# Shared sums of the second transform, mixing ahead of their reading in the drain, and an inverse root under the value products: one change to a fused attention, gated-MLP and mixer kernel

## What is computed

```
scores = q @ k.T / 8 ; thresh = max(scores) - tau
attn   = exp(scores - max), zero where scores < thresh, over its row sum
x      = attn @ v                                  (B, S, 512)

xk, xr = mu*x + (1-mu)*x_prev                      (two mixes with the row before)
k      = relu(xk @ w_k) (512->1024);  v = k*k @ w_v (1024->512)
x      = sigmoid(xr @ w_r) * v

u      = x + real(fft over channels of fft over the sequence of x)
un     = (u - mean(u)) / sqrt(var(u) + 1e-6)
out    = u + relu(un @ w_ch1) @ w_ch2              (512->2048->512)
```

## Time and profile before

| | us |
|---|---|
| median of 3 runs | 1114.38 |
| lowest, highest | 1113.59, 1114.43 |
| the profiled execution | 1115.46 |
| its span, first to last instruction | 1113.7 |

### The profile page before, as it was taken

One profiled execution on the slowest core, in us unless ns is written; L12 is line 12 of the kernel. 1 busy time (PEld: TensorE's weight loads), 2 busy tenths in 40 slices (PEclk: granted clock), 3 DMA queues, 4 the chain that ended last, 5 costly groups with the idle time before them and its releaser, 6 DMA issues.

```text
span 1113.7 us, 18462 instructions
## 1 busy us (share of the span) xinstructions
PE 1078.5 (97%) x7088; PEld 1012.4 (91%) x7088; DVE 551.7 (50%) x1081; ACT 512.7 (46%) x1250; POOL 420.0 (38%) x360
## 2 busy tenths in 40 slices
PE   7999999999999999999998999999999999999998
PEld 6899999998899998899997998888888888888998
DVE  7988764466565566565563655334114123223211
ACT  5979876646675646775644643221111111111110
POOL 5887653533663433763413445351111111111000
PEclk9989999999899999999999899999999999999999
DMA  8635111042121032121022207300200200200000
GB/s 237 176 98 170 37 43 34 24 140 53 65 56 35 23 104 89 66 57 34 2 71 77 105 1 287 122 1 1 69 1 1 69 1 1 68 1 1 35 1 33
DMA packets 37251, 69.30 MB, mean 62 GB/s; under 512 B 4134, under 2 KB 18604, under 8 KB 36140
## 3 DMA queue, kind: packets, MB, share of 16 engines
q1 hardware_dynamic: 36860, 67.80, 19.5%
q10 hardware_dynamic: 304, 0.33, 0.1%
HBM read 55.84 MB, written 12.28 MB: 61 GB/s over the span
## 4 chain that ended last, share of the span: by engine, by line
PE 82%; POOL 6%; DVE 4%; issue 3%; ACT 3%; DMA 0%; SPq 0%; DVEq 0%; POOLq 0%; ACTq 0%
PE PB L731 20%; PE PB L733 19%; PE PB L732 19%; PE PB L788 10%; PE PB L758 6%; PE PB L771 6%; POOL mix_l L630 1%; DVE probs L1284 1%; POOL x2T L662 1%; DVE neg_s L1270 1%; POOL q_hl L579 1%; POOL x2T L663 1%; POOL k_lo L571 1%; ACT exps L1019 1%; POOL fold_l L651 1%
## 5 line engine op out<-in xcount | busy, mean ns | idle before, releaser
L1228 ACT ACTIVATE h_hi<-PB 128x464 fp32r<-128x464 f32 (+1 forms) x80 | 44.5, 556 | 335.6 <-PE PB L733 335.6
L1461 DVE SCALAR_TENSOR_TENSOR h_lo<-PB,h_hi 128x464 fp32r<-128x464 f32 (+1 forms) x80 | 51.0, 638 | 264.0 <-ACT h_hi L1228 264.0
L788 PE MATMUL PB<-v_sb,probsT 128*128 128x64 f32 (+1 forms) x1440 | 180.2, 273 | 0.0
L788 PEld LDWEIGHTS PB<-v_sb,probsT 128*128 128x128 f32 x1440 | 175.1, 195 | 0.0
L1028 ACT ACTIVATE probsT<-PB 128x384 f32<-128x384 f32 (+1 forms) x288 | 109.5, 433 | 84.5 <-PE PB L771 83.5
L1284 DVE SCALAR_TENSOR_TENSOR probs<-neg_s,thresh,exps 128x576 f32<-128x576 f32 x144 | 145.7, 1012 | 0.3 <-PE PB L771 0.3
L1270 DVE TENSOR_SCALAR_CACHE_REDUCE neg_s<-PB,taus 128x576 f32<-128x576 f32 x144 | 117.1, 814 | 42.4 <-PE PB L758 38.1
L731 PE MATMUL PB<-un_h,w1h 128*128 128x464 f32 (+1 forms) x320 | 121.7, 380 | 0.0
L733 PE MATMUL PB<-un_h,w1l 128*128 128x464 f32 (+1 forms) x320 | 118.9, 371 | 0.0
L732 PE MATMUL PB<-h_lo,w2h 128*128 128x464 f32 (+1 forms) x320 | 118.8, 371 | 0.0
L731 PE MATMUL PB<-h_hi,w2h 128*128 128x464 f32 (+1 forms) x320 | 118.8, 371 | 0.0
(11 more groups left out here) (154 smaller groups left out, 2398.6 us busy)
## 6 DMA issues: line engine op xcount, KB each, us to landing
q_raw<-qT_dram SPq DMA_DIRECT2D x62, 160.0 KB, 3.2
k_raw<-kT_dram SPq DMA_DIRECT2D x64, 144.0 KB, 3.2
w_raw<-w_dram SPq DMA_DIRECT2D x8, 1024.0 KB, 9.3
cs<-cs_scr SPq DMA_DIRECT2D x4, 1740.0 KB, 8.0
u_scr<-x2T SPq DMA_DIRECT2D x4, 1152.0 KB, 5.2
cd<-cd_scr SPq DMA_DIRECT2D x4, 1032.0 KB
v_sb<-v_dram SPq DMA_DIRECT2D x16, 256.0 KB, 2.9
u_in<-u_scr SPq DMA_DIRECT2D x4, 928.0 KB, 6.1
```

Of the source, the lines that this page charges most:

```text
L788: last = nc.tensor.matmul(bank(6 + p)[:, i * DH:i * DH + width], probsT[:, n % 2, kt * P128:(kt + 1) * P128], v_sb[:, kt, pair % 2, p * DH ...
L1461: nc.vector.scalar_tensor_tensor(h_lo[:, ft % 3, 0:w], bank(4 + ft % 3)[:, 0:w], 0.0, h_hi[:, ft % 3, 0:w].bitcast(F32), ALU.max, ALU.subt ...
```

## The change

It has several parts. **(1)** The sums of tiles 1 and 2 go from POOL to DVE; POOL keeps tiles 0 and 3. The semaphore of all sums is split in two (`u_outer`, `u_inner`). **(2)** Mixing steps 4 to 7 go one slot later, and the stages after r0 take slots 13 to 34 in place of 12 to 34. **(3)** In the drain, the reading of u0/u1 and u2/u3 goes to slots 40 and 43 (39 and 41 before), all sums to slot 44, behind mixing; u3 comes behind x3 and x4 on PE, and u4 has a bank of its own. **(4)** In the first transform, the second pair of group 0 comes behind the first pair of group 1. **(5)** For dense(3): the reciprocal and Newton step go ahead of the third value group's eviction, the scaling behind the fourth, `un_l` into the second half's value stage, the low half of w_2 ahead of the last mixing steps. **(6)** POOL's split of q and k: q's low half goes ahead of k's, with q's rounding in slots 1 and 6. **(7)** `copy_head` goes one slot earlier.

```diff
-MIX_AT = [3, 4, 5, 6, 7, 8, 9, 10, 12, 13, 14, 15, 17, 18, 19, 20]
+MIX_AT = [3, 4, 5, 6, 8, 9, 10, 11, 12, 13, 14, 15, 17, 18, 19, 20]
...
-U_AT_DRAIN = [39, 39, 41, 41, 42]
+U_AT_DRAIN = [39, 39, 41, 42, 42]
...
+def u_read_at(d, pr):
+    return (40, 43)[pr] if drains(d) else U_AT[2 * pr + 1]
+def u_sum_at(d):
+    return 44 if drains(d) else U_AT[2]
...
-            return 12 + (done + i * PARTS[stage] + part) * 23 // 36
+            return 13 + (done + i * PARTS[stage] + part) * 22 // 36
...
-            order += [(d, "u", 0, 2), (d, "u", 0, 3), (d + 1, "x", 0, 3), (d + 1, "x", 0, 4), (d, "u", 0, 4)]
+            order += [(d, "u", 0, 2), (d + 1, "x", 0, 3), (d + 1, "x", 0, 4), (d, "u", 0, 3), (d, "u", 0, 4)]
...
+        elif drains(d) and stage == "u" and group[3] == 4:
+            of[group] = 4
...
+        def add_dft(engine, tile, near, far):
+            engine.tensor_tensor(x2T[:, tile, 0:NYQ], x2T[:, tile, 0:NYQ], near[:, 0:NYQ], ALU.add)
+            return engine.tensor_tensor(x2T[:, tile, NYQ:S], x2T[:, tile, NYQ:S], far[:, NYQ - 2:0:-1], ALU.add)
...
 (POOL, dense)
-                    yield u_at(d)[2]
+                    yield u_sum_at(d)
                     pool.wait_ge(ab_ready, d * 2 + 1)
-                    add_dft(0, diff[0], summ[0]).then_inc(u_part, 1)
-                    yield u_at(d)[4]
-                    pool.wait_ge(ab_ready, d * 2 + 2)
-                    add_dft(1, diff[1], summ[1])
-                    add_dft(2, summ[1], diff[1]).then_inc(u_part, 1)
-                    yield u_at(d)[4] + 1
+                    add_dft(nc.gpsimd, 0, diff[0], summ[0]).then_inc(u_outer, 1)
+                    yield u_at(d)[4] + (2 if drains(d) else 1)
                     pool.wait_ge(row_copied, d + 1)
-                    add_dft(3, summ[0], diff[0]).then_inc(u_part, 1)
+                    add_dft(nc.gpsimd, 3, summ[0], diff[0]).then_inc(u_outer, 1)
...
-                second_head = {0: (1,), 1: (2,), 2: (3, 4)}
-                next_head = {5: (1,), 6: (2,), 7: (3, 4)}
+                second_head = {0: (1,), 1: (2, 3), 2: (4,)}
+                next_head = {5: (1,), 6: (2, 3), 7: (4,)}
...
 (PE, dense)
                         first_pair(d, g)
-                        if not alone(d):
+                        if not alone(d) and g == 1:
+                            second_pair(d, 0)
+                        if not alone(d) and g >= 1:
                             second_pair(d, g)
...
 (ACT)
                         if i == 4 and d > 0:
-                            act.wait_ge(u_part, d * 3)
+                            act.wait_ge(u_inner, d)
+                            act.wait_ge(u_outer, d * 2)
...
-                                yield slot_of(d, "v", 0, 2)
+                                yield slot_of(d, "v", 0, 1, 1)
                                 root(0)
...
-                        yield u_at(d)[2 * pr + 1]
+                        yield u_read_at(d, pr)
...
-                    yield u_at(d)[4]
+                    yield u_at(d)[4] + (2 if drains(d) else 0)
                     act.wait_ge(dft_ready, d * 5 + 5)
-                    act.wait_ge(u_part, d * 3 + 1)
+                    act.wait_ge(u_outer, d * 2 + 1)
...
-                    if 0 <= n - 5 < TILES and (n - 5) % TILES_PAIR in (TAIL, TILES_PAIR - 1):
-                        copy_head(n - 5)
+                    if 0 <= n - 4 < TILES and (n - 4) % TILES_PAIR in (TAIL, TILES_PAIR - 1):
+                        copy_head(n - 4)
...
 (DVE, dense)
                                     split_w2(0, True)
-                                if alone(d) and c == 1 and ft == 0:
-                                    scale_by_rstd(0)
-                                if alone(d) and c == 1 and ft == 4:
-                                    dve.wait_ge(unh_ready, 1)
-                                    nc.vector.tensor_tensor(un_l[0][:, :, :], cent[:, :, :], un_h[0][:, :, :].bitcast(F32), ALU.subtract).then_inc(unl_ready, 1)
+                                    split_w2(0, False)
...
                                 if alone(d) and c == 0:
-                                    if i == 0:
-                                        split_w2(0, False)
-                                    if i == 2:
+                                    if i == 1:
                                         var_eps(0)
-                                    if i == 3:
                                         inverse_root(0)
                                         newton(0)
+                                    if i == 3:
+                                        scale_by_rstd(0)
+                                if alone(d) and c == 1 and i == 0:
+                                    dve.wait_ge(unh_ready, 1)
+                                    nc.vector.tensor_tensor(un_l[0][:, :, :], cent[:, :, :], un_h[0][:, :, :].bitcast(F32), ALU.subtract).then_inc(unl_ready, 1)
...
                         nc.vector.tensor_tensor(summ[pr][:, :], cos, q_cp[pr][:, :], ALU.add).then_inc(ab_ready, 1)
+                    yield u_sum_at(d) + (0 if drains(d) else 1)
+                    dve.wait_ge(ab_ready, d * 2 + 2)
+                    add_dft(nc.vector, 1, diff[1], summ[1])
+                    yield u_sum_at(d) + (0 if drains(d) else 2)
+                    add_dft(nc.vector, 2, summ[1], diff[1]).then_inc(u_inner, 1)
```

28 lines of the change are left out of this document (13 added, 15 removed).

## The result

| | before | after |
|---|---|---|
| median us | 1114.41 | 1102.66 |
| runs, lowest to highest | 4, 1113.59 to 1115.72 | 4, 1099.60 to 1105.52 |
| the profiled execution, its span | 1115.46, 1113.7 | 1105.52, 1103.7 |

The ratio is 0.9889 with a 95% interval of 0.9863 to 0.9915: 11.75 us faster, where 16.4 were forecast. The time lies in the range put on record (1092 to 1106), and 0.7 us above the narrower one of 1093.5 to 1102 that had a chance of 0.59. The four runs of the changed kernel come in two pairs, 1099.60 and 1099.92, 1105.40 and 1105.52; the profiled one is of the slower pair, so the traces differ by 10.0 us of span.

A forecast was written before the change was run, and what follows sets the result against it. PE, busy 97% of the span, was taken as the bound, leaving idle time and lower clock to win. 5.4 + 1.6 + 1.4 + 3.4 + 2.2 + 2.4 = 16.4 us off the median gave 1098.0, range 1092 to 1106.

The forecast's parts named there:

- A: At the two full boundaries between dense stages, both 2.7 us waits for the fourth mix_l go: 5.4 us.
- D: Behind the first boundary, 280 to 300 us, the clock loss goes with the idle time: 3.4 us.
- B: copy_head a slot earlier: the three x3 transposes' waits for the last head's copy all go, 1.6 us.
- C: First transform, group 0's second pair moved later: waits for fold_l shrink at three boundaries, 1.4 us.
- E: The drain: mix_l waits within r0 go, new 3.5 us waits before k cost 1.8 us of clock; 2.2 us gained.
- F: dense(3): k_sql wait and clock behind it give 3.4 us, a new table wait takes 1.0; 2.4 us gained.
- Rival 1: The lower clock comes back elsewhere: sum only 10.4 us, time 1102 to 1107; chance 0.20.
- Rival 2: Clock losses at 60 to 80 and 580 to 600 go too, the drain has none: 1092; chance 0.13.
- Rivals 3 and 4: Fourth mix_l stays late at the boundaries, 1106.8, chance 0.05; ACT or DVE becomes the bound, 1115, chance 0.03.

The follow-up runs named there:

- only_sums: The kernel before with part 1 alone, the sums of tiles 1 and 2 on DVE: 1104.35 us.
- cs_nocopy: The changed kernel with two w_1 loads moved behind the second transform's table in dense(3), and part 7 undone: 1099.31 us.
- cs_nopair: The changed kernel with two w_1 loads moved behind the second transform's table in dense(3), and part 4 undone: 1098.85 us.
- cs_nodrain: The changed kernel with two w_1 loads moved behind dense(3)'s table, and part 3 undone except DVE's share of the sums: 1101.87 us.
- only_root: The kernel before with part 5 alone: 1114.51 us, ratio 1.0010.
- after_late: The changed kernel with two w_1 loads issued only behind the first group that uses the second transform's table: 1097.72 us.
- cs_all3: The changed kernel with two w_1 loads behind dense(3)'s table, the drain's tile 0 sum behind the second mix_l, POOL's dense(3) sum of squares a slot earlier: 1093.90 us.
- cs_var: The changed kernel with two w_1 loads behind dense(3)'s table, and POOL's first-chunk sum of squares one slot earlier: 1100.37 us.
- cs_tile0: The changed kernel with two w_1 loads behind dense(3)'s table, and POOL's tile 0 sum in the drain between the second and third mix_l: 1097.09 us.

## Why the prediction was right, and where it was not

The time lay in the range and the sign was right, but the sum was 4.6 us too good, and in the profiled run its parts differ more than that. That the total came within 4.6 is partly luck: 4.1 us of clock that no part of the change won (the last row of the table) stand against losses that the sum didn't have.

| step | forecast | by stage starts | by which run |
|---|---|---|---|
| A + D | 5.4 + 3.4 | 5.9 + 3.1 = 9.0 | after; only_sums 4.5 + 1.8 |
| B | 1.6 | 0 | cs_nocopy |
| C | 1.4 | 0 | cs_nopair |
| E | 2.2 | 2.2 | after; cs_nodrain 1.0 to 3.6 |
| F, value stage | 3.4 | 4.0 | after; only_root 3.9 |
| F, table | -1.0 | -1.5 | after, only_root |
| clock behind the table | none | -7.3 | after; gone in after_late |
| wait for the part sums | none | -1.1 | after; gone in cs_all3 |
| clock at 60 to 80, 580 to 600 | none | 2.5, 1.6 | after; both in only_sums too |

**A and D held**, A by its mechanism: POOL's fourth `mix_l` at the first boundary starts at 280.98 us (288.07 before), set by ACT's `mix_h` as forecast, and PE's first product with it at 283.26 without waiting.

```profile
280.98 0.80 POOL L644 TENSOR_TENSOR mix_l<-mix_v,mix_h 128x288 fp32r<-128x288 f32 x1 [1.45 <-ACT mix_h L1113]
```

Costing DVE's four sums at nothing was right in the changed kernel: no wait for `row_max` beside them. With part 1 alone it was not (0.7 us at each boundary). D's whole 3.4 us is less sure than its row: the clock is 1.00 at both boundaries in all twelve kernels in which the wait is gone, but only_root, with the wait in place, had 1.00 at the first as well. Without the wait no loss was seen; what the wait costs differs from run to run.

**B and C failed at the same step**, "all of it goes": an idle time in front of a wait was booked as won without asking what is late next. For B it is the copy of `xT`, which must free a bank for the last transposes, and `row_max` in the first pairs (1.6 us more, against 1.4 less at `probsT`), where I had expected the idle time to be split; for C it is POOL's own pace.

**E held in size and nearly in its working.** The chain came step for step, 13.6 us earlier by what was gained ahead of it. POOL in order of time in the changed kernel, from the fourth `mix_l`:

```profile
595.02 0.80 POOL L644 TENSOR_TENSOR mix_l<-mix_v,mix_h 128x288 fp32r<-128x288 f32 x1 [0.87 <-ACT mix_h L1113]
595.78 1.02 POOL L435 TENSOR_TENSOR x2T<-x2T,diff 128x289 f32<-128x289 f32 x1
596.77 1.02 POOL L436 TENSOR_TENSOR x2T<-x2T,summ 128x287 f32<-128x287 f32 x1
598.65 0.81 POOL L435 TENSOR_TENSOR x2T<-x2T,summ 128x289 f32<-128x289 f32 x1 [0.86 <-ACT summ L1184]
599.41 1.02 POOL L436 TENSOR_TENSOR x2T<-x2T,diff 128x287 f32<-128x287 f32 x1
```

The waits stand ahead of the first four steps of k, 3.4 us together (3.5 forecast), with the clock at 0.91 from 600 to 620 us (1.8 us forecast). The four sums take 3.87 us here, near the 3.8 I had used. The Trainium skill, "GPSIMD Engine Reference", section "Key points", says that POOL contends with DVE instructions of two SBUF inputs. The trace agrees that there is contention. The prediction had worked out 5.2 us for POOL's four by it; most of it fell on DVE, whose four sums take 3.48 us (0.90, 1.06, 1.07, 0.45) where I had 1.8:

```profile
596.06 1.06 DVE L436 TENSOR_TENSOR x2T<-x2T,summ 128x287 f32<-128x287 f32 x1
597.04 1.07 DVE L435 TENSOR_TENSOR x2T<-x2T,summ 128x289 f32<-128x289 f32 x1
598.03 0.45 DVE L436 TENSOR_TENSOR x2T<-x2T,diff 128x287 f32<-128x287 f32 x1
```

The last one, with POOL idle beside it, takes 0.45.

**F failed in its second half.** The wait for the table was foreseen ("0 to 2.1 us; I take 1.0") and is 2.0, and by the named cause, the loads of w_1, which are not done when it is issued (after_late). Two things in the step were wrong, and they are where the sum failed. "Before, 7.1 was just enough" was not so: PE waited 0.5 us for it then too, under the name `y_l`, and since PE is ready 6.7 us after the issue whatever comes earlier, every landing later than that shows as a wait. And this wait was given no price in clock, though D and E had one by the same rows. That price, 7.3 us, is more than any loss in the earlier trace rows, where 3.4 was the largest; cs_nocopy and cs_nodrain lose 5.9 us at the same place, only_root 7.4. Over ten runs of only_root, part 5 without the loads moved is worth nothing.

**The part sums** were not in the sum at all. The low half of w_2 now goes ahead of the last mixing steps on DVE (2.90 us), the third `mix_l` of that stage is late by it, and POOL's sum of squares stands behind that `mix_l` in program order. The change's part (5) names the move of w_2; I had read only its gain. cs_var and cs_all3, in which that sum of squares goes ahead, have no such wait.

**The rivals.** Rival 1 (clock comes back elsewhere, 1102 to 1107, 0.20) is what happened in the measured median, though not in the way it was worked out: D gave its full 3.4 and the loss came behind the new wait. The Trainium skill, "TensorE: Matmul & The Clock Gate", section "What's actually happening", has the watch run free of the kernel; the runs agree as far as they can show it, since the runs of one kernel are some 5.7 us apart in pairs. Rival 2's losses at 60 to 80 and 580 to 600 did go (4.1 us), both by chance: only_sums, in which no instruction of either place was moved, is without them too, and cs_var, with every part of the change, had the lower clock from 575 to 585 us and lost 3.1 us more there than the kernel before. Rivals 3 and 4 fall: no `mix_l` wait at the boundaries, and PE is 20.00 of 20 us busy in both stretches.

## What to carry to other kernels

Price every wait that a change lengthens twice, its own length and the clock behind it, and for a load that PE is close to waiting for, look at what else is on the DMA engines from its issue to its landing, ahead of it and behind it in the queue. A wait named in the profile is won only if what comes after it is not late as well: of the four waits taken up here those for `mix_l` at the boundaries and for `k_sql` were won whole, those for `x_att` and `fold_l` not at all. cs_tile0 gave 0.2 us at the next stage, where taking the next wait away as well gave 3.5 us more. When the profile's name for a wait changes from kernel to kernel and its length wanders, measure the start against each candidate: the one with a constant distance is innocent.
